# Three-stage fused kernel: the value blocks of the attention in rows of 4608 bytes, and the third to fifth weight quads prepared in another order

## The reference, cut to what matters

```python
def _attn_ref(q, k, v):                      # 4 x 8 heads, 576 tokens, 64 columns
    q_d, k_d, v_d = means of q, k, v over groups of 4 tokens
    out_up = repeat(softmax(q_d k_d^T / 8) v_d, 4)
    mask = abs(pos[:, None] - pos[None, :]) < 4
    out_local = softmax(where(mask, q k^T / 8, -1e9)) v
    return out_up + out_local

x = attn.transpose(0, 2, 1, 3).reshape(2304, 512)
h = x @ w_in                                 # 512 -> 2048
x = (h - tanh(h)) @ w_out                    # 2048 -> 512
gate, val = sigmoid(x @ w_gate), x @ w_val   # 512 -> 1536, each
return (gate * val) @ w_out2                 # 1536 -> 512
```

## Time and profile before

| | us |
|---|---|
| time, median of 3 runs | 932.12 |
| lowest and highest of them | 931.35, 934.47 |
| the profiled execution | 935.37 |
| span of the profiled execution | 933.6 |
| mean granted TensorE clock in it (1 is full) | 0.982 |

### The profile page before, as it was taken

The page is one execution under the profiler, slowest core; times in us unless marked ns, Lnnn a source line. Parts: engine busy times, 40 slices in busy tenths (PEclk is TensorE's granted clock), DMA queues, the critical chain, the costliest instruction groups (busy, mean ns, idle before and its releaser), DMA issues.

```text
span 933.6 us, 15654 instructions
## 1 busy us (share of the span) xinstructions
PE 894.9 (96%) x6056; PEld 837.6 (90%) x6056; DVE 588.9 (63%) x919; ACT 387.2 (41%) x752; POOL 294.0 (31%) x237
## 2 busy tenths in 40 slices
PE   7889987999999999999998999999999999999997
PEld 4666786999999999999997999999999999999996
DVE  7778884757865657765668556566544456544444
ACT  5667953435432325332343644454222233222221
POOL 5789946773103000020016565722200001000000
PEclk9798998999999999999999999999999999999999
DMA  8989837667564545454421777769775555565511
GB/s 234 208 182 221 229 121 296 251 242 296 195 217 157 217 156 211 160 213 157 170 91 46 284 292 280 280 281 368 280 285 206 211 205 204 205 269 203 203 45 68
DMA packets 46089, 197.01 MB, mean 211 GB/s; under 512 B 3936, under 2 KB 15552, under 8 KB 33216
## 3 DMA queue, kind: packets, MB, share of 16 engines
q1 hardware_dynamic: 41984, 166.66, 51.4%
q0 software_dynamic: 4032, 29.36, 8.3%
HBM read 139.90 MB, written 56.10 MB: 210 GB/s over the span
## 4 chain that ended last, share of the span: by engine, by line
PE 83%; DMA 4%; DVE 3%; ACT 3%; POOL 3%; issue 3%; SPq 1%; ACTq 0%; DVEq 0%
PE banks L827 43%; PE banks L899 19%; PE banks L1016 16%; DMA v_win<-in_v_dram 2%; DMA win_raw<-in_moe_w_in_dram 1%; PE banks L805 1%; DVE x_op L1368 1%; PE banks L782 1%; DMA qk<-in_k_dram 1%; ACT prob_d L1058 1%; POOL win L619 1%; POOL mid L633 1%; ACT win L1080 1%; PE banks L818 1%; PE banks L760 1%
## 5 line engine op out<-in xcount | busy, mean ns | idle before, releaser
L827 PE MATMUL banks<-x_op,pair 128*128 128x384 f32 x1512 | 276.9, 335 | 1.8 <-DVE cg_sum L1545 1.8
L827 PEld LDWEIGHTS banks<-x_op,pair 128*128 128x128 f32 x1512 | 265.2, 188 | 9.7 <-DVE cg_sum L1545 2.1
L899 PE MATMUL banks<-g_parts,mid 128*128 128x384 f32 x1152 | 228.2, 337 | 12.8 <-DVE x_all L1447 6.7
L899 PEld LDWEIGHTS banks<-g_parts,mid 128*128 128x128 f32 x1152 | 203.6, 189 | 14.7 <-DVE x_all L1450 7.7
L827 PE MATMUL banks<-x_op,win 128*128 128x384 f32 x1008 | 203.7, 337 | 2.7 <-ACT x_op L1117 1.4
L827 PEld LDWEIGHTS banks<-x_op,win 128*128 128x128 f32 x1008 | 178.3, 189 | 4.0 <-ACT x_op L1117 1.9
L1016 PE MATMUL banks<-wout,p_parts 128*128 128x512 f32 x648 | 163.6, 393 | 1.7 <-issue 1.7
L1450 DVE TENSOR_TENSOR x_all<-banks,x_all 128x384 f32<-128x384 f32 x168 | 92.6, 555 | 78.2 <-PE banks L899 77.7
L1016 PEld LDWEIGHTS banks<-wout,p_parts 128*128 128x128 f32 x648 | 120.2, 188 | 22.6 <-issue 2.1
L1570 DVE TENSOR_TENSOR x_all<-banks,x_all 128x512 f32<-128x512 f32 x90 | 62.1, 690 | 113.3 <-PE banks L1016 113.3
L1138 ACT ACTIVATE banks<-c_sum 128x384 f32<-128x384 f32 x72 | 35.2, 489 | 96.9 <-DVE c_sum L1417 52.6
(11 more groups left out here) (97 smaller groups left out, 1009.0 us busy)
## 6 DMA issues: line engine op xcount, KB each, us to landing
pair<-kept_pair SPq DMA_DIRECT2D x24, 1792.0 KB, 10.8
win<-kept_in SPq DMA_DIRECT2D x16, 1792.0 KB, 7.3
kept_pair<-pair SPq DMA_DIRECT2D x12, 1792.0 KB, 12.0
mid<-kept_mid POOLq DMA_DIRECT2D x16, 1024.0 KB, 5.1
kept_in<-win SPq DMA_DIRECT2D x7, 1792.0 KB, 5.8
wout<-kept_out POOLq DMA_DIRECT2D x12, 1024.0 KB, 11.6
kept_mid<-mid SPq DMA_DIRECT2D x7, 1024.0 KB, 6.2
kept_out<-wout SPq DMA_DIRECT2D x6, 1024.0 KB, 14.9
```

What stands on the lines that cost most here:

```text
L827: mm = pe.matmul(bk[:, 0:T], weights[:, w, p - 1, kk, :], x_op[:, p - 1, x, kk, :], start=(first and kk == 0 and a == 0), stop=(last and k ...
L899: mm = pe.matmul(bk[:, 0:T], w[:, wp, f, m * P:(m + 1) * P], g[:, gp, 2 * f + t, :], start=(f == 0 and a == 0), stop=(f == 1 and a == 2))
```

## The change

The host lays the value windows out as an input of its own, `v_windows`: per unit 70 rows of 9 x 128 float32, 4608 bytes in one piece. `load_v` becomes one transfer of 70 such rows, and PE's wait counts 16 instead of 48 for a unit. The bytes loaded for the windows stay the same.

Beside it, the preparation of weights is put in another order:

- SP: `load_raw(2)` goes out with unit 8 instead of unit 14; `load_raw(3)` stands ahead of the store `keep_win(1)`; in a quad `load_raw_mid` stands ahead of the two stores. (For 2 <= n <= 5 `load_raw(n+2)` stands at the head of the quad's group as before.)
- POOL: the four sums for quad 2 move into turns 14 and 15 of the attention loop; then in its group n stand `weight_sums(n+3)`, `plain_low(n+1)`, `weight_low(n+3)`.
- ACT: `weight_high(n+1)` stands in quad n ahead of `tanh` C11 (before: `weight_high(n+2)` behind `g_high`); `weight_high(2)` comes ahead of the first `tanh` of quad 0; `x_high(0, 2)` moves one turn forward.
- DVE: `x_low(0, 4)` ahead of `second_weight_low`.

```diff
@@ load_v
-                unit = v_flat[u * P * S:(u + 1) * P * S]
-                for w, n in ((0, 1), (1, NW - 2), (NW - 1, 1)):
-                    src = bass.AP(unit.tensor, unit.offset + FIRST_KEY[w] * P, [[P, KW], [QW * P, n], [1, P]])
-                    sp.dma_start(v_win[u % 2][:, w:w + n, :], src).then_inc(s_v[u % 2], 16)
+                sp.dma_start(v_win[u % 2][:, :, :], v_windows[u // PAIRS, u % PAIRS]).then_inc(s_v[u % 2], 16)
@@ SP
-                if u == 14:
+                if u == 8:
                     load_raw(2)
             load_raw_mid(1)
+            load_raw(3)
+            keep_win(1)
 
             sp.wait_ge(s_x, UNITS)
-            for n in range(N1):
-                if 3 <= n + 2 < Q1:
+            for n in range(1, N1):
+                if 4 <= n + 2 < Q1:
                     load_raw(n + 2)
                 elif Q1 <= n + 2 < N1:
                     load_win(n + 2)
-                if 1 <= n + 1 < Q1:
+                if n + 1 < Q1:
+                    load_raw_mid(n + 1)
                     keep_win(n + 1)
-                if 1 <= n < Q1:
+                if n < Q1:
                     keep_mid(n)
-                if 2 <= n + 1 < Q1:
-                    load_raw_mid(n + 1)
@@ POOL
-            weight_sums(2, (0, 1))
+                if t == 14:
+                    weight_sums(2, (0, 1))
+                if t == 15:
+                    weight_sums(2, (2, 3))
             x_last_sum(0)
-            weight_sums(2, (2, 3))
             weight_low(2)
             for n in range(N1):
-                if 3 <= n + 2 < Q1:
-                    weight_sums(n + 2)
-                    weight_low(n + 2)
+                if n + 3 < Q1:
+                    weight_sums(n + 3)
                 if n + 1 < Q1:
                     plain_low(n + 1)
+                if n + 3 < Q1:
+                    weight_low(n + 3)
@@ PE, local_values
-                pe.wait_ge(s_v[u % 2], 48 * (u // 2 + 1))
+                pe.wait_ge(s_v[u % 2], 16 * (u // 2 + 1))
@@ ACT, first_quad
+                if 3 <= n + 1 < Q1:
+                    weight_high(n + 1)
                 tanh(n, C11)
...
                 tanh(n, C22)
                 g_high(n, 0)
-                if 3 <= n + 2 < Q1:
-                    weight_high(n + 2)
@@ ACT, attention and quad 0
                 if t == UNITS:
                     copy_c(0, C11)
-                    x_high(0, 2)
                     x_high(0, 5)
                 if t == UNITS + 1:
                     x_high(0, 4)
+
+                    act.wait_ge(s_vd, UNITS)
+                    weight_high(2)
                     tanh(0, C11)
...
+                if t == UNITS - 1:
+                    x_high(0, 2)
...
-
-            act.wait_ge(s_vd, UNITS)
-            weight_high(2)
             plain_high(1)
@@ DVE
+            x_low(0, 4)
             second_weight_low()
-            x_low(0, 4)
@@ host
+        if name == "v":
+
+            first = [min(max(64 * w - 3, 0), s - 70) for w in range(s // 64)]
+            a = _np.ascontiguousarray(_np.stack([a[:, :, f:f + 70, :] for f in first], axis=3))
```

3 lines of the change are left out of this document (added).

## The result

The changed kernel takes 927.22 us, median of five runs (925.44 to 927.93), where the kernel before takes 933.87 beside it: ratio 0.9931, 95% interval 0.9911 to 0.9952. So it is faster by 6.7 us, or 0.7%, and not by the 20.8 us forecast. Measured again on two other chips the ratio was 0.9931 (0.9897 to 0.9964) and 0.9933 (0.9910 to 0.9957). Executions more than 1.5% above the fastest of their kernel are left out of every median, ratio and profile here.

The account below looks back on a forecast made before the run. It took attention to be bound by DMA in its first half and POOL in its second. From the median 932.12 us, 7 + 1 + 9.0 + 3.8 = 20.8 us gave 911, range 903 to 923 (about 0.86).

Parts of the forecast that it names:

- Windows in one piece: Attention up to unit 7, about 60 us: larger window pieces relieve DMA and give 7 us, bounds 0 to 9.2.
- 252 GB/s: Full DMA rate at 16 to 20 us, against 206 from 20 to 60; gave up to 1.15 us a unit.
- POOL's idle time, 13.5 us: Four POOL waits before about 51 us, 3.40 + 1.78 + 2.23 + 6.05, as the most the windows could win.
- the windows give nothing: Rival for attention: 512-byte pieces don't slow the DMA, the 7 us stay away, 918 us; chance 0.15.
- The end of attention: Quad 2's sums ahead of POOL's last normalisings, `x_low(0, 4)` earlier on DVE: net gain 1 us, bounds -2 and +3.
- The first gap: PE's gap of 6.68 us before 147.82 and 2.3 us of clock loss behind it go: 9.0 us.
- The second: PE's gap of 1.89 us before 198.78 and 1.9 us of clock loss behind it go: 3.8 us.
- Slack 4 us, and so have quads 4 to 7, each shifted by 15.6: `weight_low(3)` ends 4 us before quad 3's first product needs it; quads 4 to 7 likewise, 15.6 us apart.
- From quad 8 on: The rest of the program from quad 8 should be unchanged to within 1 us.
- ACT's `weight_high`: Ahead of `tanh` C11 it fills an ACT wait: price 0, or up to 1.7 us a quad, five quads.
- `load_raw(2)`: At unit 8 its 512 KB stand ahead of the next units' loads: price 0, bounds 0 to 2.2 us.
- the rival of DVE and POOL blocking each other: In the quads, `g_low` beside POOL's work costs time: 920 to 929 chance 0.13, about 930 chance 0.02; slower 939.

Follow-up runs that it names:

- e6_no_windows: Changed kernel with the window loads of units 2 to 15 left out, so its values are not the reference's: 918.22 us, ratio 0.9861 to the kernel before.
- e10_one_transfer_512: Changed kernel, quad 7's raw load earlier, quad 2's sums behind the attention loop, quad 1's first sums at turn 6, windows one transfer of 512-byte packets: 922.85 us.
- e4_sums_after: Changed kernel with the four sums for quad 2's weights behind the attention loop again: 920.12 us, ratio 0.9875 to the kernel before.
- e3_mid_first: Changed kernel with quad 7's raw load ahead of the store `keep_mid(5)` and the load of quad 8: 923.04 us, ratio 0.9910 to the kernel before.
- e1_windows_only: Kernel before with only the windows' layout changed, one transfer of 4608-byte rows a unit: 931.65 us, ratio 1.0019 to the kernel before.
- e2_order_only: Changed kernel with the three small window loads a unit of the kernel before, new order kept: 923.92 us, ratio 0.9926 to the kernel before.
- e5_sums1_later: Changed kernel with the first two sums for quad 1's weights at POOL's turn 6 instead of 5: 922.83 us, ratio 0.9905 to the kernel before.
- e7_again: Repeat of changed kernel with quad 7's raw load earlier, quad 2's sums behind the attention loop, quad 1's first sums at turn 6: 918.72 us, ratio 0.9867.

## Why the prediction was wrong

The direction and both gaps were right, the size was not: 6.7 us instead of 20.8, outside the range.

*Windows in one piece: 7 forecast, 0 measured.* This is the step that failed. Four pairs of kernels that differ in the layout alone stand at +0.7, +0.9, +0.3 and -1.5 us, new against old. Three things were wrong in it.

First, the rate. The 252 GB/s were to be the speed "while no windows were yet on the way". The DMA packets of 16 to 20 us in the profile before say otherwise:

```profile
DMA packets 744, 0.92 MB, mean 229 GB/s; under 512 B 55, under 2 KB 418, under 8 KB 743
```

418 - 55 = 363 of the 744 packets have 512 bytes, and in this program only the windows have such. So the 2.4 us a unit, and the 1.15 us that each was to give back, rest on a comparison of windows with windows; the rival's "as high before windows came in" falls with it. The packets themselves give less. From 20 to 110 us a packet of 512 bytes took 46 ns in the profile before and a row of 4608 took 274 in the one after, so a unit's windows fill the 16 DMA engines for 630 x 46 / 16 = 1.8 us and 70 x 274 / 16 = 1.2 us: 0.6 us saved. In five other profiles of the old layout the packet took 39 to 41 ns, which makes it about 0.4 us or less.

Second, the prize. "POOL's idle time, 13.5 us" came from an execution that was 4.9 and 7.1 us later at unit 6 than the other two of its kernel. I had its distance to the median in hand, 3.3 us, and took it off the total, not off the stretch where it lay. (The list of four waits was also short by two, 3.60 us for a value block before 6.33 us and 3.42 for DVE before 11.81.)

Third, the path. A faster queue only ends one of several waits: in the table of the profiles above, what POOL no longer waits for DMA it waits for PE and DVE. `e6_no_windows` sets about 6.5 us as the worth of all the bytes. The rival "the windows give nothing" had this right. It leaned on the figure of 512 bytes in the Trainium skill, "DMA: Bandwidth & Descriptors", section Specifications, which I had set aside for two rows. The traces agree with the rule, nearly: 512 bytes took 35 ns as a packet of one large transfer (`e10_one_transfer_512`), and 274 / 9 = 30 ns within a row of 4608. The rival's 918 us was too low all the same: 7 of its 13.8 us were lost at other places.

*The end of attention: +1 forecast with -2 as its bound, -3.1 measured.* The delay of POOL's last normalising by the four sums was priced (2.9); that the first two sums hold up unit 14's as well, so that PE has nothing to do for 2.22 us, was not, and neither was the half clock behind it. I had priced this very clock loss at the two gaps and not asked where the change makes a new one. `e4_sums_after` has neither, and its median is 4.7 us lower. Where the half clock stayed short, in `e3_mid_first`, this stretch took 76.7 us against 77.4 to 78.2 before: there the forecast gain of 1 us is seen.

*The first gap: 9.0 forecast, 7.9 measured. The second: 3.8 forecast, 3.8 measured.* Both steps hold; PE has no gap from 127 to 217 us, at a clock of 1.00. (The first gap counts as measured with whatever else changed in quads 0 and 1.)

*"Slack 4 us, and so have quads 4 to 7, each shifted by 15.6": -3.5 measured.* True of the weights up to quad 6, wrong at quad 7. The cure of the second gap, `x_sums` behind `weight_low(6)`, had no price: POOL waits 5.66 us there for ACT, so the x sums and with them `plain_low(5)` come late, and so does the store `keep_mid(5)`. And I took `load_raw_mid` to come "only earlier", though SyncE's list has it behind that store and now right behind the 1.8 MB of `load_win(8)`. `e3_mid_first` shows the second part.

*From quad 8 on "unchanged within 1 us": -1.7.* At the change of stage the granted clock is 0.66 in 498 to 503 us of the first profile after, 1.00 there before. `e1_windows_only`, which has the old order, loses 2.1 us there too, and `e2_order_only`, `e5_sums1_later`, `e6_no_windows` and `e7_again` lose nothing. So neither half of the change decides it alone; what does isn't shown.

*ACT's `weight_high`, `load_raw(2)`, the rival of DVE and POOL blocking each other:* none of them opens a gap in the early quads. So of all the terms one came out as forecast and one nearly, and every other one lower.

## What to carry to other kernels

Before pricing a wait that DMA ends, look at how its kernel's runs scatter and at where the profiled one lies: a stretch that varies by 5 us from run to run can't carry a term of 7. Before taking a stretch as the one "without" some traffic, count its packets by size. Relieving one of several waits that end within a microsecond or two of one another hands the time to the next; leaving the traffic out altogether is the test for the upper bound. Where work is moved ahead of something that TensorE waits for, price the pause and then the half clock behind it, and follow each queue to its head past every wait that stands in it.

## What the runs showed of the hardware

TensorE stopped in the middle of a row of matmuls without waits for up to 4.05 us, with the DMA engines nearly full and a packet of 16,384 bytes of the instruction queue under way; the profile calls it "issue". In ten runs of one unchanged kernel the time went roughly with the granted clock, 919.13 us at 0.991 to 931.67 at 0.978. A pause of 2.2 to 2.3 us went with 13.6 to 13.7 us at 1.2 GHz in three profiles and with 3.4 us in two others. In the first profile after, TensorE was never idle in the 12 us from its return at 107.49 us on (the stretches of 108 to 120 us are full), and still ran at 1.2 GHz.
